# A fused attention, feed-forward and routing kernel: narrow fp32 products for the logits, and work moved between engines

## The reference, cut to what matters

```python
state = gamma * state + outer(k[t], v[t]);  y[t] = q[t] @ state / 8     # 4 batches, 8 heads, 768 steps, 64 wide
x = y as (3072, 512)
r = maximum(x @ w_in, 0);  g = s * r * r + b                           # w_in 512 x 2048
x2 = g @ w_out                                                          # w_out 2048 x 512
logits = x2 @ w_gate                                                    # 8 experts
# tokens go to experts in falling order of the flattened logits, each expert takes at most 384
out[mask_e] = maximum(x2[mask_e] @ w1[e], 0) @ w2[e]                    # w1 512 x 1024, w2 1024 x 512
```

## Time and profile before

| | |
|---|---|
| median of three runs | 953.67 us (953.37 to 955.79) |
| the profiled execution | 955.8 us, of which its span is 953.5 us |
| TensorE busy | 936.2 us, 98% of the span |
| VectorE busy | 512.6 us, 54% |
| ScalarE busy | 295.9 us, 31% |
| GpSimd busy | 239.2 us, 25% |
| one relu on ScalarE (L737), mean | 599 ns |
| one square, one low half of g on VectorE (L1262, L1266), mean | 820 ns, 824 ns |
| one low half of w_in in block 0 (L1215 VectorE, L640 GpSimd), mean | 711 ns, 1361 ns |
| DMA | 193.50 MB, 203 GB/s on average |
| up phase on TensorE | from 24.18 us to about 372 us |
| last tile of the down phase | from 652.93 us, experts from 670.44 us |

### The profile page before, as it was taken

One profiled execution on the slowest core, in us unless ns is written; L12 is line 12 of the kernel. 1 busy time (PEld: TensorE's weight loads), 2 busy tenths in 40 slices (PEclk: granted clock), 3 DMA queues, 4 the chain that ended last, 5 costly groups with the idle time before them and its releaser, 6 DMA issues.

```text
span 953.5 us, 18333 instructions
## 1 busy us (share of the span) xinstructions
PE 936.2 (98%) x7364; PEld 755.7 (79%) x7364; DVE 512.6 (54%) x1172; ACT 295.9 (31%) x552; POOL 239.2 (25%) x224
## 2 busy tenths in 40 slices
PE   7999999999999999999999999999999999999997
PEld 5776777877777777777777777777898998998996
DVE  4755555665665555567766766772544344434420
ACT  2443434434433453010101010100443443534521
POOL 4532122231232000001111111001435534643611
PEclk9999999999999999999999999999999999999999
DMA  8895566566665477757675767284636446535500
GB/s 307 314 346 207 194 236 243 219 222 227 239 233 211 162 249 265 284 183 234 202 235 188 244 196 243 78 256 152 221 100 209 157 133 199 180 127 180 177 34 33
DMA packets 81411, 193.50 MB, mean 203 GB/s; under 512 B 8880, under 2 KB 17456, under 8 KB 81328
## 3 DMA queue, kind: packets, MB, share of 16 engines
q1 hardware_dynamic: 77488, 179.76, 55.7%
q0 software_dynamic: 3840, 12.59, 4.0%
HBM read 129.14 MB, written 63.18 MB: 202 GB/s over the span
## 4 chain that ended last, share of the span: by engine, by line
PE 94%; DVE 1%; DMA 1%; SPq 1%; issue 1%; ACT 0%; POOLq 0%; POOL 0%; DVEq 0%
PE bank L1037 28%; PE bank L1142 27%; PE bank L1183 14%; PE bank L1198 14%; PE bank L988 3%; PE bank L899 1%; PE bank L858 1%; PE bank L1163 1%; PE bank L887 1%; PE bank L1068 1%; PE bank L923 1%; DMA early_qT<-in_q_turned 1%; PE bank L1001 1%; PE bank L1093 1%; DMA g_late<-g_rows 0%
## 5 line engine op out<-in xcount | busy, mean ns | idle before, releaser
L1037 PE MATMUL bank<-x,wi_hi 128*128 128x512 f32 x768 | 242.4, 397 | 1.3 <-DVE x L1256 1.3
L1037 PEld LDWEIGHTS bank<-x,wi_hi 128*128 128x128 f32 x768 | 141.0, 188 | 52.6 <-issue 16.4
L695 POOL TENSOR_TENSOR w_lo<-w_raw,w_hi 128x512 fp32r<-128x512 f32 x72 | 94.8, 1324 | 292.9 <-ACT w_hi L804 292.7
L1262 DVE SCALAR_TENSOR_TENSOR u_sb<-u_sb,cst 128x512 f32<-128x512 f32 x96 | 78.7, 820 | 145.6 <-ACT u_sb L737 145.4
L1037 PE MATMUL bank<-x,wi_lo 128*128 128x512 f32 x384 | 149.7, 390 | 0.0
L1142 PE MATMUL bank<-wo_b,g_back 128*128 128x512 f32 x552 | 137.9, 400 | 0.0
L804 ACT ACTIVATE w_hi<-w_raw 128x512 fp32r<-128x512 f32 x128 | 76.5, 638 | 166.8 <-DMA w_raw<-in_w 166.5
L737 ACT ACTIVATE u_sb<-bank 128x512 f32<-128x512 f32 x96 | 57.5, 599 | 194.3 <-PE bank L1037 194.3
L1142 PEld LDWEIGHTS bank<-wo_b,g_back 128*128 128x128 f32 x552 | 99.4, 189 | 18.6 <-issue 0.8
L1544 DVE TENSOR_TENSOR w_lo<-w_raw,w_hi 128x512 fp32r<-128x512 f32 x56 | 60.8, 1085 | 68.2 <-ACT w_hi L804 67.5
L1183 PE MATMUL bank<-xg_hi,w_hi 128*128 128x384 f32 x256 | 86.8, 339 | 0.0
(11 more groups left out here) (196 smaller groups left out, 1208.3 us busy)
## 6 DMA issues: line engine op xcount, KB each, us to landing
g_rows<-g_sb SPq DMA_DIRECT2D x96, 512.0 KB, 3.0
g_back<-g_rows SPq DMA_DIRECT2D x80, 512.0 KB, 4.2
w_raw<-in_w SPq DMA_DIRECT2D x128, 256.0 KB, 3.7
x_rows<-x SPq DMA_DIRECT2D x25, 256.0 KB, 5.1
g_back<-g_rows SPq DMA_DIRECT2D x16, 384.0 KB, 4.4
kT<-in_k_turned SPq DMA_DIRECT2D x22, 256.0 KB, 4.0
qT<-in_q_turned SPq DMA_DIRECT2D x22, 256.0 KB, 4.1
vin<-in_v SPq DMA_DIRECT2D x22, 256.0 KB, 4.2
```

The costliest lines, as they stand in the source:

```text
L695: pool.tensor_tensor(low, w_raw[:, (p * E_PIECES + n) % RAW, :], high.bitcast(F32), ALU.subtract).then_inc(w1_lo_done, 1)
L1037: last = pe.matmul(up[i % 2][:, :], w[:, t, fs], x[:, half, t, :], start=(t == 0 and n_ == 0), stop=(t == DT - 1 and n_ == 2))
L1262: dve.scalar_tensor_tensor(u, u, sc_s, u, ALU.mult, ALU.mult).then_inc(u_done, 1)
```

## The change

Five things are changed together.

1. `w_og_turn` and `logits` make each 128-column fp32 product as four products with 32 stationary columns each, which go to four groups of 32 output partitions and so to four column groups of the array. 4 products become 16. This holds for the 4 quarters of w_og and for the 6 blocks.
2. The steps of the w_og quarters move. The first `w_og_parts` goes from after f = 5 to after f = 2, its turn from f = 6 to f = 3, the first quad from f = 7 to f = 4; the turns of the others now come right behind an insert or a quad. `logits(blk)` for blocks 0 to 4 goes from f = 4 of the next block to f = 6, behind the insert and the quad of that step. w_og's PSUM place moves from bank 4 to bank 0.
3. All low halves of w_in are made by VectorE; GpSimd makes none. Pieces 1 and 2 now stand on VectorE between `x_low(2)` and `x_low(3)`.
4. VectorE adds the new state (`add_state`) before the square of the step instead of after x_low, and the first quarter of the turned w_out and w_gate are loaded ahead of pieces 4 to 7 of w_in instead of behind piece 8.
5. Of the 16 loads of `g_late`, 12 instead of 8 are issued before the last rows of the down phase are stored; from f = 12 of the last block on, two of them per step instead of one.

The diff, without renamed semaphores and the counting functions that fall away:

```diff
-FIRST_QUAD_AT = {7: 0, 11: 1, 14: 2}
-LAST_QUAD_AT, LOGITS_AT = 2, 4
-
-W_OG_AT = {(0, 5): 0, (0, 9): 1, (0, 12): 2, (1, 0): 3}
-W_OG_TURN_AT = {(0, 6): 0, (0, 10): 1, (0, 13): 2, (1, 1): 3}
-TURNED_AT = {0: 0, 3: 1, 6: 2, 9: 3}
-BIAS_AT, CAST_AT, DIGITS_AT = (1, 3), (1, 1), (1, 4)
+FIRST_QUAD_AT = {4: 0, 11: 1, 14: 2}
+LAST_QUAD_AT, LOGITS_AT = 2, 6
...
+W_OG_PART_AT = {2: 0, 6: 1, 10: 2, 13: 3}
+W_OG_AT = {3: 0, 8: 1, 11: 2, 14: 3}
+TURNED_AT = {2: 1, 4: 2, 8: 3}
+BIAS_AT, CAST_AT, DIGITS_AT = (1, 1), (1, 1), (1, 4)
...
-POOL_LOWS = (1, 2, 4, 5, 8, 10, 12, 14)
...
+LATE_LOAD_AT = {8: (0,), 9: (1,), 10: (2,), 11: (3,), 12: (4, 5), 13: (6, 7), 14: (8, 9), 15: (10, 11)}
...
-        w_og_part, w_og_ps, bias_ps = bank[3], bank[4][:, 0:4 * EXPERTS], bank[0][:, 320:320 + EXPERTS]
+        w_og_part = bank[3]
+        w_og_ps, bias_ps = bank[0][:, 384:384 + 4 * EXPERTS], bank[0][:, 320:320 + EXPERTS]
...
             load("kin", 3)
             load_chunk(4)
+            sp.dma_start(wg[:, :, :].rearrange("p t e -> p (t e)"), w_gate).then_inc(gate_in, 16)
+            load_turned(0)
             for i in range(STAGE, 2 * STAGE):
                 load_piece(i)
             load_chunk(5)
             sp.dma_start(cst[:, N_EARLY:], const[:, N_EARLY:]).then_inc(const_in, 16)
-            sp.dma_start(wg[:, :, :].rearrange("p t e -> p (t e)"), w_gate).then_inc(gate_in, 16)
-
...
-                if blk == N_BLK - 1 and f >= LOADS:
-                    load_late(f - LOADS)
+                if blk == N_BLK - 1:
+                    for late in LATE_LOAD_AT.get(f, ()):
+                        load_late(late)
             for tile in range(TILES - CPB, LATE):
                 store_row(tile)
-            for f in range(FT - LOADS, FT):
+            for f in range(1 + max(sum(LATE_LOAD_AT.values(), ())), FT):
...
-            def piece(i):
-                pool.wait_ge(piece_hi, i + 1)
-                _, hi, lo = piece_at(i)
-                pool.tensor_tensor(lo, staging[:, i % STAGE, :], hi.bitcast(F32), ALU.subtract).then_inc(piece_lo_pool, 1)
-
             decay_k(0)
...
-            piece(1)
-            piece(2)
             decay_k(CPB - 1)
             decay_k(CPB)
-            piece(4)
-            piece(5)
...
-                if n == CPB + 1:
-                    piece(10)
-                if n == CPB + 2:
-                    piece(14)
                 age_state(n + 1)
                 decay_k(n + 1)
-                if n == CPB:
-                    piece(8)
-                if n == CPB + 1:
-                    piece(12)
...
-                    if (blk, f) in W_OG_AT:
-                        w_og_copy(W_OG_AT[blk, f])
                     if (blk, f) in WO_AT:
                         piece(WO_AT[blk, f])
+                    if blk == 0 and f in W_OG_PART_AT:
+                        w_og_copy(W_OG_PART_AT[f])
...
                     if (blk, f) == CAST_AT:
                         act.wait_ge(const_in, 16)
+                        act.wait_ge(w_og_done, QUADS)
...
-                if CPB + 1 < n <= CPB + 1 + QUADS:
-                    pe.wait_ge(w_og_copied, n - CPB - 1)
-                    pe.wait_ge(w_og_ready, n - CPB - 1)
+                if CPB < n <= 2 * CPB + 1:
+                    pe.wait_ge(w_og_ready, max(n - CPB - 1, 1))
+                    pe.wait_ge(w_og_copied, min(n - CPB, QUADS))
...
             def w_og_parts(c):
-                if c == 0:
-                    pe.wait_ge(gate_in, 16)
+
+                pe.wait_ge(gate_in, 16)
                 pe.wait_ge(turned_in[c], 16)
-                pe.wait_ge(att_masked, 2 * (CPB + c + 2))
+                pe.wait_ge(att_masked, 2 * (CPB + c + 1))
                 for t in range(DT):
                     last = pe.matmul(w_og_part[32 * t:32 * (t + 1), :], wg[:, t, :],
                                      w_turned[:, t, c * HALF:(c + 1) * HALF], start=True, stop=True, skip_group_check=True)
                 last.then_inc(w_og_parted, 1)
 
             def w_og_turn(c):
+
                 pe.wait_ge(w_og_copied, c + 1)
-                if c == 0:
-                    pe.wait_ge(const_in, 16)
-                pe.wait_ge(state_added, adds(CPB + c + 2))
+                pe.wait_ge(const_in, 16)
+                pe.wait_ge(state_added, adds(CPB + 1 + c if c else CPB) + 1)
                 for j in range(4):
-                    f = 4 * c + j
-                    last = pe.matmul(w_og_ps[:, j * EXPERTS:(j + 1) * EXPERTS], w_turned[:, 0, f * P:(f + 1) * P], sel,
-                                     start=True, stop=True)
...
+                    for m in range(4):
+                        at = (4 * c + j) * P + 32 * m
+                        last = pe.matmul(w_og_ps[32 * m:32 * (m + 1), j * EXPERTS:(j + 1) * EXPERTS],
+                                         w_turned[:, 0, at:at + 32], sel, start=True, stop=True, skip_group_check=True)
+                last.then_inc(w_og_done, 1)
...
-                n = (blk + 2) * CPB + 1
+                n = (blk + 2) * CPB + 2
                 pe.wait_ge(state_added, adds(n) + 1 if n < TILES else adds(TILES))
                 if blk:
...
                 else:
                     pe.wait_ge(bias_ready, 1)
+                pe.wait_ge(const_in, 16)
                 for c in range(CPB):
-                    last = pe.matmul(logit_ps(blk)[:, c * EXPERTS:(c + 1) * EXPERTS], partial[:, c * P:(c + 1) * P], sel,
-                                     start=True, stop=True)
+                    for m in range(4):
+                        at = c * P + 32 * m
+                        last = pe.matmul(logit_ps(blk)[32 * m:32 * (m + 1), c * EXPERTS:(c + 1) * EXPERTS],
+                                         partial[:, at:at + 32], sel, start=True, stop=True, skip_group_check=True)
...
                     if f in ATT_AT[blk]:
                         if blk and f > LOGITS_AT:
                             pe.wait_ge(logit_copied, blk)
+                        if blk == 1 and f == min(ATT_AT[1]):
+                            pe.wait_ge(bias_ready, 1)
                         insert((blk + 1) * CPB + ATT_AT[blk][f])
-                    if (blk, f) in W_OG_AT:
-                        w_og_parts(W_OG_AT[blk, f])
-                    if (blk, f) in W_OG_TURN_AT:
-                        w_og_turn(W_OG_TURN_AT[blk, f])
                     quads = QUAD_AT if blk else FIRST_QUAD_AT
                     if f in quads:
                         quad(blk, quads[f])
+                    if blk == 0 and f in W_OG_PART_AT:
+                        w_og_parts(W_OG_PART_AT[f])
+                    if blk == 0 and f in W_OG_AT:
+                        w_og_turn(W_OG_AT[f])
...
                 if n == CPB - 2:
                     piece(0)
                 x_low(n)
+                if n == CPB - 2:
+                    piece(1)
+                    piece(2)
             piece(3)
...
             for blk in range(N_BLK):
                 for f in range(FT):
                     i = blk * FT + f
+                    if (blk, f) == (1, 0):
+                        bias_total()
+                    if f in ATT_AT[blk] and (blk + 1) * CPB + ATT_AT[blk][f] + 1 < TILES:
+                        add_state((blk + 1) * CPB + ATT_AT[blk][f] + 1)
                     square(i)
                     if i:
                         g_low(i - 1)
                     if blk == 0 and f in WI_AT:
                         for j in WI_AT[f]:
-                            if j not in POOL_LOWS:
-                                piece(j)
+                            piece(j)
                     if (blk, f) in WO_AT:
...
-                    if (blk, f) in W_OG_TURN_AT:
-                        w_og_copy(W_OG_TURN_AT[blk, f])
+                    if blk == 0 and f == min(W_OG_AT):
+                        w_og_copy(0)
...
                         n = (blk + 1) * CPB + ATT_AT[blk][f]
                         x_low(n)
                         if n + 1 < TILES:
-                            add_state(n + 1)
                             mask(n + 1)
+                        if blk == 0 and f in W_OG_AT:
+                            w_og_copy(W_OG_AT[f])
```

43 lines of the change are left out of this document (17 added, 26 removed).

## The result

The changed kernel takes 944.62 us (median of four runs, 944.06 to 947.43) against 953.72 (953.37 to 955.79): a ratio of 0.9906, 95% interval 0.9882 to 0.993. The profiled execution took 947.43 us with a span of 945.4, so some 8 us less span than before.

The account below looks back on a forecast made before the run. TensorE, busy 98% of the span, was taken to bound the kernel. Gains and losses of 4.0 + 1.45 + 0.66 - 0.2 - 0.2 = 5.7 us gave 953.67 - 5.7 = 948.0 us for the median, range 945.2 to 951.4.

Parts of the forecast that it names:

- the price of a group: Turns and logits on TensorE: 32 narrow instructions would take 0.46 us, 14.4 ns each, where a group cost 0.90 us.
- ten groups: Four w_og turns and six logits blocks, made with narrow products, would together gain 4.0 us.
- wait of the first parts: TensorE's wait for VectorE's mask before the first w_og parts would go, gaining 1.45 us.
- late loads, last tile: With fewer g_late loads behind the row stores, a 0.66 us wait at the last tile would go.
- wait for the w_og copy: Behind the first turn, TensorE would wait for VectorE's copy before increment(5): 0.2 us lost, from 0 to 1.5.
- x_low(3) behind two low halves: Low halves of pieces 1 and 2 on VectorE would delay the first up product: 0.2 us lost, 0 to 0.5.
- The floor: Rival, chance 0.13: TensorE can't start small products closer than 25 ns, so 0.80 us per group; kernel 951.4 us.
- the dearer products: Rival, chance 0.06: narrow products at 50 ns, 1.60 us per turn or logits group; kernel 5.9 us slower, 959.6.
- VectorE behind: Rival, chance 0.07: w_og copy 1.5 us late, masks or low halves of f = 8 another 1; kernel 950.3 us.
- The 0.34: Last tile: 0.34 us lost before the 25th product was to reappear as waiting for gathered rows, which the stores set.
- My bound of 1.2: Upper end, in us, of the gain expected from earlier g_late loads, if the gather comes earlier too.
- my upper bound of 0.5: Largest loss expected, in us, from two low halves at 0.92 each ahead of x_low(3) on VectorE.

## Why the prediction was wrong

It had the mechanism, the places and the direction right, and mis-sized three terms of the sum; the price of a group is the one that counts. The range was set narrower than its own bounds, too: the best of them together gave 944.8, and I began it at 945.2. In us:

| term | predicted | measured |
|---|---|---|
| ten groups | 4.0 | 5.7 |
| first quad now beside an insert | not counted | 0.2 |
| wait of the first parts | 1.45 | 1.5 (2.84 to 1.32) |
| late loads, last tile | 0.66 | 1.4 (17.51 to 16.13) |
| wait for the w_og copy | -0.2 | 0 |
| x_low(3) behind two low halves | -0.2 | -0.7, and at times the clock |

*The price of a group* is the step that failed: "as many instructions and as many tiles, so I take 0.46 us per group". Per instruction that is 14.4 ns; it is 8.4 (the changed profile, and 0.28 to 0.30 for 32 in the run with doubled groups). The insert streams and loads 64 columns and works on two column tiles by two row tiles; the new form has 32 and 8, and four column tiles. The row that was like it in columns and tiles, the loads of a quad at 7.4 ns, I had used as the bound only. Which of the differences makes the insert dearer is not shown. With their exits the ten groups cost 0.56 (first turn), 0.44, 0.36 (in the run with one late load per step, since a stall lies in this insert here), 0.37, five times 0.27 and 0.47 (last logits): 3.6 us against 9.3 before, of which the first logits group had 1.09 and not 0.90, which I had not looked at.

*The floor and the dearer products* were rivals. 21 ns for four in a row on one tile shows that something near the floor is real where neighbours share their columns, and that the order of the two loops decides it; the 60 cycles of overhead that the Trainium skill gives for each matmul ("TensorEngine Tiling (Array Packing)", section "Instruction Overhead") do not hold across column tiles, where it is 8.4 ns.

*VectorE behind* did not happen. The copy of w_og was done ahead of the increment that waits for it:

```profile
42.61 0.18 DVE L1269 COPY w_og<-bank 128x32 f32<-128x32 f32 x1
```

```profile
43.53 0.58 PE L865 MATMUL bank<-vin,kin 64*64 64x64 f32 x14
```

*Late loads.* "The 0.34 only moves into the wait for the gathered rows" was wrong: the rows came in time, and both waits for g_late went. Of the 1.4 us, 0.5 lie in the first 24 products, 0.2 in the next twelve, 0.6 behind the turn. My bound of 1.2 was too low too: it was made of the waits of one execution, and the wait of 1.54 us with one load per step shows how they vary. That the rows come in time is not safe either: with all groups wide TensorE waited 0.98 us for them.

*x_low(3).* "Two low halves at 0.6 fit into that gap to the tenth" held in two profiles of six. In the others my upper bound of 0.5 was too low: two low halves beside GpSimd's early_kin took 2.04 us, one of them 1.44, where I took 0.92 as the worst. That the delay of 0.7 us can cost the clock too was in no term.

*GpSimd* was in no term ("nobody waits longer for it"), and TensorE waited 1.1 us for its kin in the profile after; the instruction stall of the profile before, 0.75 at 73 us, is not in this one, so the two nearly cancel. Two smaller slips changed nothing: the 16 of the earlier trace rows are instructions, so eight products, and full DMA engines move 380 to 400 GB/s (windows above), not 308.

The measured terms add up to 8.1 us, and the spans differ by 8.0. This is partly chance: some 0.7 us of the shorter up phase I can't assign, and the profile after began 0.7 us later than the profile before. The last attention product begins at 22.52 against 21.81, because the first mask waited longer for its load (VectorE began it at 9.33 and 8.69, behind `DMA att_decay<-in_decays`). The change has no part in that: in eight variants of the changed kernel this product begins at 19.8 to 21.1 us, in three of the kernel before at 20.1, 20.2 and 21.7. From it to the end it takes 931.6 us before and 922.9 after, 8.7 less, which is nearer to the 9.1 between the medians. Both profiled executions began later than most of the others, and they lie above their medians, by 2.1 and 2.8 us.

## What to carry to other kernels

Small products of which each goes to another 32 columns of the array than the one before follow each other at 8.4 ns, the same products in a row on one tile at 21 ns, 128-wide ones at 100 ns (each per instruction, two to a product): order them so, and put them behind other tiled work. Take the price of a new form from the row with the same columns and tiles, not from the one with the same instruction count. A wait of TensorE of 2 us or more may cost its length and 1.7 us of lost clock again, unless a later wait takes that up; keep low halves, or anything else, out of VectorE's queue ahead of what TensorE waits for, above all where a GpSimd instruction may begin just before them. Where a wait has no name, look at what the code waits for there and at the queue of instructions, before calling it a stall. Compare profiles from a point behind their starts.
